# Moving the sums and roundings of Strassen operands T1 to T4 earlier at the batch boundaries of a fused attention and feed-forward kernel

## Chip, cores and metric

The kernel runs as one program on 1 core of a Trainium2 chip. The metric is its device time in microseconds, as the median of several runs; a lower time is better.

## What is computed

The reference is a linear attention, followed by two feed-forward layers. The change touches the first of them, `h = x @ w_in`, and what stands around it.

```python
# attention: q, k, v of (8 batches, 8 heads, 576 tokens, 64)
q_s = np.exp(q - np.max(q, axis=-1, keepdims=True))
q_s = q_s / (np.sum(q_s, axis=-1, keepdims=True) + 1e-09)
k_s = np.exp(k - np.max(k, axis=2, keepdims=True))
k_s = k_s / (np.sum(k_s, axis=2, keepdims=True) + 1e-09)
kv = np.einsum('bhsd,bhse->bhde', k_s, v)
x = np.einsum('bhsd,bhde->bhse', q_s, kv)        # then (4608 tokens, 512)
# first layer: w_in (512, 2048), w_out (2048, 512)
r = np.maximum(x @ w_in, 0.0)
x = (r * r) @ w_out
# second layer: rms norm, silu(xn @ w_gate) * (xn @ w_val) @ w_out
```

## The kernel before

**Products.** Every fp32 product is made of three matmuls in TensorE's round fp32 format: an operand is split in a rounded part ("hi", ScalarE, line 1116) and the rest ("lo", VectorE, line 1423, which reads the operand and its hi part). TensorE multiplies hi by hi, lo by hi and hi by lo (lines 1797 to 1799). The product `x @ w_in` of one batch (576 tokens, in two halves of 288) is a Strassen product: 7 products in place of 8. The four blocks of x are B11, B21 (first half of the tokens), B12, B22; the sums are T1 = B12 - B11, T2 = B22 - T1, T3 = B22 - B12 and T4 = B21 - T2. The seven operands of a batch are B11, T2, T1, B21, T3, T4, B22. GpSimd makes the sums: T1 at line 894 and T2 at line 899; T3 at line 902; T4 in two instructions, at lines 906 and 908, which overwrite the place in `xa` where T1 stands (so they wait until T1 is split). Batch 0 alone is computed as a plain product of four blocks; batches 1 to 7 go the Strassen way.

**Quads.** A batch has 8 quads (a quad is a pair of output blocks of 128 columns, times the two halves of the tokens), and a quad takes 7 steps on TensorE, one product (6 matmuls of 128x288) each. The order of the steps is B11, T2, T1, B21, then T4 and B22 of the quad before, then T3. All quads of a batch read the same seven operands in `TAR`, so operands are made once per batch, around the boundary between two batches. The tile `TAR` has 9 entries, so that most operands of a batch are written while those of the batch before are still read.

**Evacuation.** ScalarE copies the first product's bank (`h_copy_p1`, line 1157); TensorE adds B21 into that bank only after this copy (`pe.wait_ge(hp1_done, n)`). VectorE makes the other blocks: line 1471 (`h_u2`, which needs the copy, and for which T3 waits), 1476 (`h_21`), 1482 (`h_12`; the T1 product of the next quad but one waits for it), 1487 and 1489 (`h_22`).

**Attention beside it.** While a batch goes through the first layer, the attention of the next batch is computed in 4 units (c = 0 to 3), each a row of small tasks: `qmax` (VectorE, 1363), `qsub` (GpSimd, 882), `qexp` (ScalarE, 1070), `qsum` and `qinv` (VectorE, 1366 to 1373), `qnorm` (GpSimd, 885), then transposes of q (TensorE, 1786), the kv product (1771) and the x product (1790), with copies out of the banks by ScalarE (1086, 1090); kexp is at 1067, and kmax at 1358.

**The order.** Every engine runs its own list in order, with semaphore waits. The lists come from tables: `UNIT_*` give the steps of the attention's tasks, and `add_batches` adds, for each batch, splits and sums at step `start_of(b) + n - 56`, so n = 56 is the first step of batch b and n = 49 is the first step of the last quad of the batch before. Within a step the attention's tasks come first. The first unit of the batch after next to be computed has `qmax` at step 52, `qsub` and `kmax` at 53, `qexp` at 55, `qsum` at 56 and `qnorm` at 58 by the same count. The batch 7 boundary has no unit, since there is no batch 8.

```python
def ta_split(b, i):            # VectorE
    dve.wait_ge(ta_hi, split_a(b, i))
...
    if m == 0:                 # TensorE, the first quad of a batch
        pe.wait_ge(ta_lo, split_a(b, i))
...
elif which == T4 (the last branch of xa_sums, GpSimd):
    pool.wait_ge(ta_lo, split_a(b, T1))
```

`split_a` counts splits in the order of `SPLIT_A`.

Of the kernel before, what the change touches and what calls it, by code (L numbers as in the profile page):

```python
# [30 lines left out]
B11, T2, T1, B21, T3, T4, B22 = range(7)  # L31
# [20 lines left out]
NQA = B * PA  # L52
H_SETS = 3
W1_ALONE = 3
SPLIT_A = (B11, T2, T1, B21, T3, T4, B22)
SPLIT_PLAIN = (B11, B12, B21, B22)
PLAIN_ENTRY = {B11: 3, B12: 4, B21: 5, B22: 6}
BLOCKS = ((B11, B21), (B12, B22))
# [6 lines left out]
def start_of(b):  # L65
    return STEPS_PLAIN + STEPS * (b - 1) if b else 0
# [6 lines left out]
def split_a(b, i):  # L73
    return 4 + 7 * (b - 1) + SPLIT_A.index(i) + 1 if b else SPLIT_PLAIN.index(i) + 1

# [43 lines left out]
def unit_table(events):  # L119
    table = {}  # L120
    for b in range(1, B):
        for c in range(KC):
            base = start_of(b - 1) + UNIT_BASE[b - 1][c]
            for what, n in events:
                table.setdefault(max(0, base + n), []).append((what, b, c))
    return table


PE_AT, DVE_AT, ACT_AT, POOL_AT, SP_AT = (unit_table(t) for t in (UNIT_PE, UNIT_DVE, UNIT_ACT, UNIT_POOL, UNIT_SP))


def add_batches(table, what, at, second, later):
    for b in range(1, B):
        for i, n in at + (second if b == 1 else later):
            table.setdefault(start_of(b) + n - STEPS, []).append((what, b, i))


add_batches(ACT_AT, "split", [(B11, 28), (T2, 49), (T1, 51), (B21, 52), (T3, 55)], [(T4, 62), (B22, 64)], [(T4, 60), (B22, 63)])
add_batches(DVE_AT, "split", [(B11, 29), (T2, 50), (T1, 52), (B21, 53), (T3, 57)], [(T4, 64), (B22, 66)], [(T4, 62), (B22, 65)])
add_batches(POOL_AT, "sum", [(T1, 30), (T2, 47), (T3, 51)], [(T4, 60)], [(T4, 57)])  # L140
for _m in range(2, PA):
    ACT_AT.setdefault(8 * _m - 9, []).append(("w1", 0, _m))
    DVE_AT.setdefault(8 * _m - 8, []).append(("w1", 0, _m))
# [1930 lines left out]
```

## Time and profile before

| | |
|---|---|
| median of 3 runs | 1681.9 us (1679.25 to 1682.57) |
| the profiled execution | 1681.12 us |
| its span, first to last instruction | 1679.4 us |
| granted TensorE clock | 0.999 |
| TensorE busy (matmul) | 1652.1 us, 98% |
| VectorE busy | 1162.4 us, 69% |
| ScalarE busy | 615.1 us, 37% |
| GpSimd busy | 592.1 us, 35% |
| DMA queue's share of 16 engines | 41.6% |

The engines are called PE (TensorE), DVE (VectorE), ACT (ScalarE) and POOL (GpSimd) in the profile. A busy share is a mean over stages; what a stage is limited by is read from who waits for whom in that stage. The first Strassen layer lies between about 91 and 484 us, and its batches repeat every 56.4 us.

### The profile page before, as it was taken

The page shows a single profiled execution, that of the slowest core. Times are in us where ns is not written, and L with a number is a line of the kernel's source. Part 1 is how long each engine was busy: PE and PEld are TensorE (multiplying, and loading weights), DVE is VectorE, ACT ScalarE, POOL GpSimd, SP SyncE. Part 2 cuts the span into 40 slices and gives each one's busy share as a digit, 9 for nine tenths or more (in the row PEclk, how much of TensorE's full clock was granted, in tenths as well). Part 3 has the DMA queues.
Part 4 walks back from the last instruction along what each step waited for, and adds up shares of the span by engine and source line. Part 5 has one row for each costly group of instructions (what it writes and reads, how often), then busy time and mean ns, then how long its engine had stood idle before and what let it go on. Part 6 is the DMA issues. An engine that isn't in the chain of part 4 may idle for free.

```text
span 1679.4 us, 26396 instructions
## 1 busy us (share of the span) xinstructions
PE 1652.1 (98%) x9926; PEld 1510.5 (90%) x9926; DVE 1162.4 (69%) x1749; ACT 615.1 (37%) x1056; POOL 592.1 (35%) x470
## 2 busy tenths in 40 slices
PE   7999999999999999999999999999999998999999
PEld 6999999999988888888888988988998988999999
DVE  6687667667566778787776565546555568877775
ACT  5544334333232323333334432323332334343432
POOL 3553323332102224342256744546455553000000
PEclk9999999999999999999999999999999999999999
DMA  8665545554463454444432322242321334434441
GB/s 260 211 227 172 172 160 185 172 163 152 144 219 88 125 170 119 119 120 126 119 126 88 113 88 107 83 138 82 110 88 67 110 127 164 141 132 151 147 139 56
DMA packets 151742, 230.06 MB, mean 137 GB/s; under 512 B 11840, under 2 KB 75840, under 8 KB 151616
## 3 DMA queue, kind: packets, MB, share of 16 engines
q1 hardware_dynamic: 151616, 228.38, 41.6%
q8 instruction: 80, 1.31, 0.3%
q14 instruction: 46, 0.38, 0.1%
HBM read 143.39 MB, written 84.93 MB: 136 GB/s over the span
## 4 chain that ended last, share of the span: by engine, by line
PE 87%; DVE 6%; POOL 3%; DMA 2%; issue 1%; ACT 1%; SPq 0%; DVEq 0%; POOLq 0%; ACTq 0%
PE bank L1797 14%; PE bank L1798 14%; PE bank L1799 14%; PE bank L1883 7%; PE bank L1885 7%; PE bank L1884 7%; PE bank L1973 5%; PE bank L1975 5%; PE bank L1974 5%; PE bank L1771 2%; PE bank L1790 2%; DVE TAR L1423 1%; PE bank L1786 1%; DMA h_scratch<-hb 1%; PE bank L1818 1%
## 5 line engine op out<-in xcount | busy, mean ns | idle before, releaser
L1797 PE MATMUL bank<-TR,SW 128*128 128x512 f32 (+1 forms) x840 | 309.0, 368 | 0.3 <-DVE TR L1538 0.3
L1799 PE MATMUL bank<-TR,SW 128*128 128x512 f32 (+1 forms) x840 | 309.1, 368 | 0.0
L1798 PE MATMUL bank<-TR,SW 128*128 128x512 f32 (+1 forms) x840 | 309.1, 368 | 0.0
L1797 PE MATMUL bank<-TAR,SA 128*128 128x288 f32 x784 | 250.7, 320 | 5.5 <-DVE TAR L1423 2.8
L1798 PE MATMUL bank<-TAR,SA 128*128 128x288 f32 x784 | 231.5, 295 | 0.0
L1799 PE MATMUL bank<-TAR,SA 128*128 128x288 f32 x784 | 231.0, 295 | 0.0
L1883 PE MATMUL bank<-GH,W 128*128 128x512 f32 x576 | 224.7, 390 | 2.0 <-DVE GH L1443 2.0
L1885 PE MATMUL bank<-GH,W 128*128 128x512 f32 x576 | 224.5, 390 | 0.0
L1884 PE MATMUL bank<-GH,W 128*128 128x512 f32 x576 | 224.5, 390 | 0.0
L1132 ACT ACTIVATE GH<-g 128x512 fp32r<-128x512 f32 x144 | 91.2, 634 | 244.6 <-DVE g L1438 159.5
L1975 PE MATMUL bank<-SW,OA 128*128 128x256 f32 x630 | 179.3, 285 | 0.0
L1973 PE MATMUL bank<-SW,OA 128*128 128x256 f32 x630 | 179.3, 285 | 0.0
L1974 PE MATMUL bank<-SW,OA 128*128 128x256 f32 x630 | 179.3, 285 | 0.0
L1797 PEld LDWEIGHTS bank<-TR,SW 128*128 128x128 f32 x840 | 157.8, 188 | 20.5 <-DVE TR L1538 0.6
L1798 PEld LDWEIGHTS bank<-TR,SW 128*128 128x128 f32 x840 | 157.8, 188 | 19.8
L1799 PEld LDWEIGHTS bank<-TR,SW 128*128 128x128 f32 x840 | 157.8, 188 | 19.6
L1443 DVE TENSOR_TENSOR GH<-g,GH 128x512 fp32r<-128x512 f32 x144 | 138.7, 963 | 40.7 <-ACT GH L1132 40.6
L1797 PEld LDWEIGHTS bank<-TAR,SA 128*128 128x128 f32 x784 | 147.6, 188 | 10.5 <-DVE TAR L1423 4.6
L1798 PEld LDWEIGHTS bank<-TAR,SA 128*128 128x128 f32 x784 | 147.9, 189 | 2.5
L1799 PEld LDWEIGHTS bank<-TAR,SA 128*128 128x128 f32 x784 | 147.5, 188 | 0.0
L1013 POOL TENSOR_TENSOR group<-group,group 128x512 f32<-128x512 f32 (+1 forms) x60 | 73.0, 1216 | 189.9 <-DVE group L1584 189.5
L1883 PEld LDWEIGHTS bank<-GH,W 128*128 128x128 f32 x576 | 108.2, 188 | 25.1 <-DVE GH L1443 2.7
(176 smaller groups left out, 3344.0 us busy)
## 6 DMA issues: line engine op xcount, KB each, us to landing
h_scratch<-hb SPq DMA_DIRECT2D x128, 288.0 KB, 2.7
hst<-h_scratch SPq DMA_DIRECT2D x144, 256.0 KB, 2.7
araw<-a_scratch SPq DMA_DIRECT2D x18, 1536.0 KB, 6.8
a_scratch<-group SPq DMA_DIRECT2D x72, 256.0 KB, 2.0
xst<-xn_scratch SPq DMA_DIRECT2D x10, 1024.0 KB, 5.1
xn_scratch<-x SPq DMA_DIRECT2D x9, 1024.0 KB, 5.4
a_scratch<-group SPq DMA_DIRECT2D x48, 192.0 KB, 1.9
out<-ost SPq DMA_DIRECT2D x36, 256.0 KB, 2.0
```

The source lines that it names most:

```text
L1013: nc.gpsimd.tensor_tensor(a1, a1, val1, ALU.mult).then_inc(a1_done, 1)
L1132: nc.scalar.activation(GH[:, r % GH_RING, 0], g[:, r % G_RING], ACT.Copy).then_inc(ghi_done, 1)
L1443: nc.vector.tensor_tensor(GH[:, r % GH_RING, 1], g[:, r % G_RING], f(GH[:, r % GH_RING, 0]), ALU.subtract)\
L1797: nc.tensor.matmul(ps[:, 0:w], w_hi[:, cc], x_hi[:, c], start=opens and c == 0, stop=False, skip_group_check=True)
L1798: nc.tensor.matmul(ps[:, 0:w], w_lo[:, cc], x_hi[:, c], start=False, stop=False, skip_group_check=True)
L1799: last = nc.tensor.matmul(ps[:, 0:w], w_hi[:, cc], x_lo[:, c], start=False, stop=c == 1, skip_group_check=True)
L1883: nc.tensor.matmul(acc[c][:, :], W2[:, j, 0, cc], GH[:, r % GH_RING, 0], start=j == 0, stop=False, skip_group_check=True)
L1884: nc.tensor.matmul(acc[c][:, :], W2[:, j, 1, cc], GH[:, r % GH_RING, 0], start=False, stop=False, skip_group_check=True)
L1885: last = nc.tensor.matmul(acc[c][:, :], W2[:, j, 0, cc], GH[:, r % GH_RING, 1], start=False, stop=j == CA - 1, skip_group_check=True)
L1973: nc.tensor.matmul(ps, a_hi, w_hi, start=start, stop=False, skip_group_check=True)
L1974: nc.tensor.matmul(ps, a_lo, w_hi, start=False, stop=False, skip_group_check=True)
L1975: last = nc.tensor.matmul(ps, a_hi, w_lo, start=False, stop=stop, skip_group_check=True)
```

## The change

Three table lines and the tuple `SPLIT_A` change. T1 is split before T2 instead of after it. T4's two sums come directly behind T3's sum on GpSimd, ahead of the next unit's `qsub`; before, they came behind it. T3 and T4 are split at steps 53 and 54 of the old batch (ScalarE) and 54 and 55 (VectorE); before, at 55 and 60 (62 for batch 1), and 57 and 62 (64). No instruction is added or removed.

```diff
-SPLIT_A = (B11, T2, T1, B21, T3, T4, B22)
+SPLIT_A = (B11, T1, T2, B21, T3, T4, B22)
...
-add_batches(ACT_AT, "split", [(B11, 28), (T2, 49), (T1, 51), (B21, 52), (T3, 55)], [(T4, 62), (B22, 64)], [(T4, 60), (B22, 63)])
-add_batches(DVE_AT, "split", [(B11, 29), (T2, 50), (T1, 52), (B21, 53), (T3, 57)], [(T4, 64), (B22, 66)], [(T4, 62), (B22, 65)])
-add_batches(POOL_AT, "sum", [(T1, 30), (T2, 47), (T3, 51)], [(T4, 60)], [(T4, 57)])
+add_batches(ACT_AT, "split", [(B11, 28), (T1, 49), (T2, 51), (B21, 52), (T3, 53), (T4, 54)], [(B22, 64)], [(B22, 63)])
+add_batches(DVE_AT, "split", [(B11, 29), (T1, 50), (T2, 52), (B21, 53), (T3, 54), (T4, 55)], [(B22, 66)], [(B22, 65)])
+add_batches(POOL_AT, "sum", [(T1, 30), (T2, 47), (T3, 51), (T4, 52)], [], [])
```

GpSimd at the boundary to batch 2, before: T2's sum, T3's sum, `qsub`, T4's two sums, `qnorm`.

```order
L899 TENSOR_TENSOR TAR_106<-xa 128x576
L902 TENSOR_TENSOR xa<-xa 128x2x288
L882 TENSOR_TENSOR qn_113<-qn_113,qmax 128x640
L906 TENSOR_TENSOR xa<-xa 128x2x288
L908 TENSOR_TENSOR xa<-xa 128x2x288
L885 TENSOR_TENSOR qn_113<-qn_113,qinv 128x640
```

The same place after the change:

```order
L899 TENSOR_TENSOR TAR_106<-xa 128x576
L902 TENSOR_TENSOR xa<-xa 128x2x288
L906 TENSOR_TENSOR xa<-xa 128x2x288
L908 TENSOR_TENSOR xa<-xa 128x2x288
L882 TENSOR_TENSOR qn_113<-qn_113,qmax 128x640
L885 TENSOR_TENSOR qn_113<-qn_113,qinv 128x640
```

`qsub` (882) now stands behind both of T4's sums.

ScalarE at the same boundary, before: the evacuation copy of the old batch's last quad (1157), the splits of T2 (`TAR_106`) and T1, `h_11` (1164), the split of B21, `qexp` (1070), the split of T3, then the copy of the new batch's first quad, and the split of T4 behind `h_11`.

```order
L1157 ACTIVATE hb_0_126<-bank 128x288
L1116 ACTIVATE TAR<-TAR_106 128x576
L1116 ACTIVATE TAR<-xa 128x576
L1164 ACTIVATE hb_0_125<-bank 128x288
L1116 ACTIVATE TAR<-xa 128x576
L1070 ACTIVATE qn_113<-qn_113 128x640
L1116 ACTIVATE TAR<-xa 128x576
L1157 ACTIVATE hb_1_128<-bank 128x288
L1164 ACTIVATE hb_1_127<-bank 128x288
L1116 ACTIVATE TAR<-xa 128x576
```

After the change (the row with x3 is B21, T3 and T4):

```order
L1157 ACTIVATE hb_0_126<-bank 128x288
L1116 ACTIVATE TAR<-xa 128x576
L1116 ACTIVATE TAR<-TAR_106 128x576
L1164 ACTIVATE hb_0_125<-bank 128x288
L1116 ACTIVATE TAR<-xa 128x576 x3
L1070 ACTIVATE qn_113<-qn_113 128x640
L1157 ACTIVATE hb_1_128<-bank 128x288
L1164 ACTIVATE hb_1_127<-bank 128x288
```

T4's split now stands ahead of `qexp` and of the copy of the new batch's first quad.

VectorE from `kmax` (1358) of the same boundary to `h_u2` (1471) of the new batch's first quad and the rows behind it, before:

```order
L1358 TENSOR_REDUCE kmax<-kT_111 128x1
L1423 TENSOR_TENSOR TAR<-xa,TAR 128x576
L1482 TENSOR_TENSOR hb_2_129<-hb_2_129,bank 128x288
L1487 TENSOR_TENSOR hb_0_126<-hb_0_126,bank 128x288
L1489 TENSOR_TENSOR hb_0_126<-hb_0_126,bank 128x288
L1366 TENSOR_REDUCE qden<-qn_113 128x10
L1369 TENSOR_SCALAR qden<-qden 128x10
L1373 RECIPROCAL qinv<-qden 128x10
L1471 TENSOR_TENSOR hb_1_127<-hb_1_128,bank 128x288
L1423 TENSOR_TENSOR TAR<-xa,TAR 128x576
```

After the change:

```order
L1358 TENSOR_REDUCE kmax<-kT_111 128x1
L1423 TENSOR_TENSOR TAR<-xa,TAR 128x576
L1482 TENSOR_TENSOR hb_2_129<-hb_2_129,bank 128x288
L1423 TENSOR_TENSOR TAR<-xa,TAR 128x576
L1487 TENSOR_TENSOR hb_0_126<-hb_0_126,bank 128x288
L1489 TENSOR_TENSOR hb_0_126<-hb_0_126,bank 128x288
L1423 TENSOR_TENSOR TAR<-xa,TAR 128x576
L1366 TENSOR_REDUCE qden<-qn_113 128x10
L1369 TENSOR_SCALAR qden<-qden 128x10
L1373 RECIPROCAL qinv<-qden 128x10
L1471 TENSOR_TENSOR hb_1_127<-hb_1_128,bank 128x288
```

The lo splits of T3 and T4 moved from behind `h_u2` to ahead of `qsum` (1366) and `h_u2`.

## Rows read from the trace of the kernel before

**Rows 1.** The page's part 1: busy time, share and instructions by engine.

```profile
PE 1652.1 (98%) x9926; PEld 1510.5 (90%) x9926; DVE 1162.4 (69%) x1749; ACT 615.1 (37%) x1056; POOL 592.1 (35%) x470
```

**Rows 2.** Waits of PE: total us, times, longest us.

```profile
PE bank L1797 <- DVE TAR L1423: 2.8, 6, 0.5
```

**Rows 3.** Timeline of PE, boundary to batch 2: start, duration, [idle before <-releaser].

```profile
150.14 0.30 PE L1797 MATMUL bank<-TAR,SA 128*128 128x288 f32 x1
...
152.52 0.29 PE L1799 MATMUL bank<-TAR,SA 128*128 128x288 f32 x1
153.30 0.40 PE L1797 MATMUL bank<-TAR,SA 128*128 128x288 f32 x1 [0.49 <-DVE TAR L1423]
153.53 0.29 PE L1798 MATMUL bank<-TAR,SA 128*128 128x288 f32 x1
...
154.19 0.49 PE L1786 MATMUL bank<-ident,qn 128*128 128x128 f32 x3
```

**Rows 4.** Timeline of DVE, boundary to batch 2.

```profile
144.31 0.75 DVE L1423 TENSOR_TENSOR TAR<-TAR,TAR 128x576 fp32r<-128x576 f32 x1
...
145.71 0.75 DVE L1423 TENSOR_TENSOR TAR<-xa,TAR 128x576 fp32r<-128x576 f32 x1
146.38 0.45 DVE L1476 TENSOR_TENSOR hb<-hb,bank 128x288 f32<-128x288 f32 x1
146.74 0.74 DVE L1358 TENSOR_REDUCE kmax<-kT 128x1 f32<-128x576 f32 x1
147.41 0.79 DVE L1423 TENSOR_TENSOR TAR<-xa,TAR 128x576 fp32r<-128x576 f32 x1
...
149.34 0.81 DVE L1366 TENSOR_REDUCE qden<-qn 128x10 f32<-128x640 f32 x1
150.18 0.85 DVE L1369 TENSOR_SCALAR qden<-qden 128x10 f32<-128x10 f32 x1
...
151.20 0.43 DVE L1471 TENSOR_TENSOR hb<-hb,bank 128x288 f32<-128x288 f32 x1
151.55 1.69 DVE L1423 TENSOR_TENSOR TAR<-xa,TAR 128x576 fp32r<-128x576 f32 x1
```

**Rows 5.** Timeline of POOL, boundary to batch 2.

```profile
142.63 1.45 POOL L902 TENSOR_TENSOR xa<-xa 128x576 f32<-128x576 f32 x1
145.87 1.71 POOL L882 TENSOR_TENSOR qn<-qn,qmax 128x640 f32<-128x640 f32 x1 [1.79 <-DVE qmax L1363]
147.54 1.95 POOL L906 TENSOR_TENSOR xa<-xa 128x576 f32<-128x576 f32 x1
149.57 1.44 POOL L908 TENSOR_TENSOR xa<-xa 128x576 f32<-128x576 f32 x1
151.37 1.26 POOL L885 TENSOR_TENSOR qn<-qn,qinv 128x640 f32<-128x640 f32 x1 [0.36 <-DVE qinv L1373]
```

**Rows 6.** Timeline of ACT, boundary to batch 2.

```profile
147.62 0.74 ACT L1070 ACTIVATE qn<-qn 128x640 f32<-128x640 f32 x1 [1.09 <-POOL qn L882]
148.26 0.67 ACT L1116 ACTIVATE TAR<-xa 128x576 fp32r<-128x576 f32 x1
148.84 0.39 ACT L1157 ACTIVATE hb<-bank 128x288 f32<-128x288 f32 x1
```

**Rows 7.** Timeline of DVE, boundary to batch 1, and the stretch behind it.

```profile
92.89 0.17 DVE L1369 TENSOR_SCALAR qden<-qden 128x10 f32<-128x10 f32 x1
...
93.27 0.45 DVE L1471 TENSOR_TENSOR hb<-hb,bank 128x288 f32<-128x288 f32 x1
...
101.92 1.44 DVE L1423 TENSOR_TENSOR TAR<-xa,TAR 128x576 fp32r<-128x576 f32 x1
```

**Rows 8.** Timeline of PE behind the boundary to batch 1.

```profile
99.50 1.39 PE L1771 MATMUL bank<-vn,kt 128*128 128x129 f32 x10 [0.97 <-ACT qT L1086]
...
102.97 0.29 PE L1799 MATMUL bank<-TAR,SA 128*128 128x288 f32 x1
...
103.66 0.29 PE L1798 MATMUL bank<-TAR,SA 128*128 128x288 f32 x1
```

## The prediction

> **What bounds the kernel now.** I read the page first: TensorE is busy 98% of the span [rows 1], so only an idle stretch of TensorE can be won, and every new one is paid in full. The waits of PE come next. In the first layer the wait that this change can touch is the T3 product's for VectorE's lo split: 2.8 us in 6 waits [rows 2], one at each boundary to batches 1 to 6. Then the timelines of one boundary. PE's rows show what one wait costs: matmuls start every 0.13 us, so after 152.52 the second one of T3 was due at 152.78; it starts at 153.53, so 0.75 us is lost, 0.49 of it shown as idle [rows 3]. VectorE's rows show why: T3's lo split takes 1.69 us instead of 0.75 [rows 4], because `qnorm` runs on GpSimd from 151.37 to 152.63 [rows 5]. The split ends 0.61 us behind that.
>
> **The port rule that the rest uses.** An instruction of GpSimd and a lo split of VectorE do not run together. A split that meets a running GpSimd instruction ends 0.61 us after it (151.37 + 1.26 = 152.63; 151.55 + 1.69 = 153.24) [rows 4, 5]. A GpSimd instruction that meets a running split waits until about 0.64 us after the split's start: T4's first sum takes 1.95 instead of 1.44, so it truly begins at 148.05, against the split's start at 147.41 [rows 4, 5]. A split that had to wait frees the other 0.47 behind the instruction it waited for (I take 0.14 less than its end, as in the undisturbed one). VectorE's evacuations and reductions keep their durations beside GpSimd.
>
> The Trainium skill, page "SBUF — State Buffer", section "SBUF: two separate sides", says the same in sharper form: a VectorE operation with two SBUF inputs and a GpSimd operation that reads SBUF exclude each other, the first to start holds the port pair for its whole instruction. By that rule the pair would come free at 148.20 instead of 148.05; the row decides for the earlier release.
>
> **What the change removes.** T3's split moves ahead of `qnorm`, so the 0.75 us wait loses its cause at five boundaries (batches 2 to 6).
>
> **What it adds.** GpSimd runs T4's sums ahead of `qsub`, and ScalarE has T4's split, which waits for those sums, ahead of `qexp`, and both ahead of `h_copy_p1` of the new batch's first quad. TensorE's B21 product waits for that copy. I work the chain out for batch 2; up to the first lateness TensorE stands where it stands now.
>
> - T1's lo split takes the place of T2's: 144.31 to 145.06 [rows 4].
> - T4's first sum: 0.08 behind it (the gap between the two sums, 149.49 to 149.57), 145.14 to 146.59. T3's sum ended at 144.08, so GpSimd is free [rows 5].
> - T2's lo split starts at 145.71 [rows 4], meets this sum, and ends at 147.20, freeing the port at 147.06.
> - T4's second sum: due 146.67, begins at 147.06, ends at 148.50.
> - VectorE's next start is 147.13, 0.07 ahead of the end; 0.36 for line 1476 and 0.67 for `kmax` [rows 4] bring B21's lo split to 148.16. It meets the second sum, ends at 149.11, frees the port at 148.97.
> - `qsub`: 148.97 plus 1.26. That is its undisturbed duration (1.71 less the 0.45 during which the split of 145.71 held the port) [rows 4, 5]. It ends at 150.23.
> - `qexp`: 0.04 later, 150.27; the next ScalarE instruction starts 0.64 after it [rows 6], so the copy runs 150.91 to 151.32. Before it started at 148.84 [rows 6].
> - B21's first matmul was at 150.14 [rows 3]. Now 0.06 behind the copy, 151.38; the second follows a restart after 0.23, as at 153.30 to 153.53 [rows 3]: 151.61 against 150.27, so **1.34 us** is lost. The smaller lateness in front of it (`h_12` ends at 149.48, T1's product due at 149.34) lies inside this.
>
> What is late next: the `h_u2` for T3's product. VectorE after B21's split: `h_12` from 149.04, T3's split from 149.40. It meets `qsub`, which ends at 150.23, and so ends at 150.84. `h_22` (two instructions, 0.86 by starts: 149.34 less 147.41 is 1.93, less 0.71 for a split and 0.36) from 150.77; T4's split 151.63 to 152.38; `qsum` from 152.30 (0.84 to the next start, 149.34 to 150.18) [rows 4]; from line 1369 to `h_u2` 0.38, as 92.89 to 93.27 where nothing disturbs it [rows 7]. `h_u2` runs 153.52 to 153.97. T3's first matmul is at 154.03, the second at 154.26 against 152.78: **1.48 us** lost in all. Then `qnorm`, started 0.08 behind `qinv`'s end at 153.57, ends at 154.91; the transposes of q, which follow T3's first matmul by 0.89 (153.30 to 154.19) [rows 3], are due at 154.92. They come 0.05 to 0.15 late. I take 0.1: 1.58 us.
>
> **The sum.** At boundaries 2 to 6: 1.58 lost instead of 0.75, five times 0.83 = +4.2 us.
> At boundary 1 the same chain makes T3's product about 1.1 us later than before, but TensorE then waits 0.97 us for the copy of q [rows 8], which was late because T4's split stood ahead of it on ScalarE and waited for T4's sums. That wait goes as the other comes: taken together 0. B22's split (1.44 us [rows 7]) meets no `qsub` there any more, since the T4 sums no longer stand ahead on GpSimd; the product B22 lost 103.66 less 102.97 less 0.27 = 0.42 [rows 8]. So -0.4.
> At boundary 7 there is no unit, hence no `qsub` and no `qexp`: the copy would come 1.26 + 0.04 + 0.64 = 1.94 earlier than the 151.32 of the same place, at 149.38, which is ahead of 150.14. So 0.
> Total +3.8 us. The profiled execution took 1681.12 with a span of 1679.4; its span would be 1683.2. The median of before, 1681.9, is 0.8 above the profiled execution; with the same sum on it I predict **1685.7 us**. All later stages are as before, and move with TensorE. No DMA changes its place in SP's queue; at boundary 1 one store waits some 3 us longer for VectorE's copy, with loads behind it that are needed over 10 us later. I cost it at nothing.
>
> **Bounds.** From below: no sum meets a split. Then the sums end at 148.11, `qsub` at 149.30, the copy at 150.39, B21's second matmul at 150.68: 0.41 lost, 0.34 less than now, -1.7 us for five. With all that boundary 1 can give (0.97 + 0.42 = 1.4) it is -3.1: 1678.8. From above: each hold lasts the whole 0.75, three of them on the way to `qsub`, 0.42 a boundary, 2.1 in all, and boundary 1 gives nothing: 3.8 + 2.1 + 0.4 = +6.3: 1688.2. I stay with the release that the rows show.
>
> **Rivals.**
> - *The new wait is about as long as the old one.* For it: the port rule rests on few rows, and who gets the port first at 148.50 is not certain; any of the meetings at 145.71, 148.16 and 149.40 may fall away by a shift of some tenths. Result between -1.7 and +2.5 us, 1680.2 to 1684.4, about 1682.
> - *Faster.* T3's wait goes, and nothing takes its place: the copy at boundaries 2 to 6 ends before 150.08. It decides at `qsub`: this must end by 150.08 - 0.41 - 0.64 - 0.04 = 148.99. Against it: T4's two sums and `qsub`, 1.45 + 0.08 + 1.44 + 1.26 less 0.07 of overlap, take 4.16 us from 145.14 even without any meeting, and end at 149.30. For it: spans on GpSimd are rough, and 0.31 is little. Price: 5 x 0.75 + 1.4 = 5.1 us, 1676.8.
> - *The port is held longer*, or the late `h_u2` makes later quads late too (`h_12` and `h_21` of the old batch's last quad follow it on VectorE): 0.42 more a boundary, 1687.8. Against it: T4's split is no longer in the way there, and the rows of before have idle VectorE soon after. By the page's rule the whole instruction holds the pair, which is this case; the trace shows an earlier release.
>
> **How the numbers follow.** A measurement of this kernel can tell about 0.2%, 3.4 us, from no change. Forecast, +2.5 to +5.5: 0.52, of which 0.35 above +3.4. New wait like the old: 0.20. Faster: 0.13 (1676.8, or less of it, but past -3.4). Longer hold: 0.15. Slower by over 0.2% is 0.35 + 0.15 = 0.50; within, 0.17 + 0.20 = 0.37; faster 0.13. The range 1678.8 to 1688.5 takes in both bounds and leaves out most of the faster case and the tail above.
>
> **What would show it.** In the profile of the changed kernel: no wait of line 1797 for TAR's lo split at boundaries 2 to 6; in its place a wait of the B21 product for line 1157, about 1 us each, and one of some tenths for line 1471 or 885. `qexp` at 150.3 by the same clock, ScalarE idle ahead of T4's split for line 908. At boundary 1 no wait of line 1771 for qT. The period of batches 57.3 us instead of 56.4. Wrong would be: `qsub` ending near 149.3 (no meetings at the port), or a wait of T2's or B21's product for its split, which I have as on time by 1.3 and 1.0 us.

## The result, and the profile after

The changed kernel takes 1685.47 us (median of 12 runs, 1684.47 to 1686.70), the kernel before 1681.76 us in runs beside it (median of 12). The ratio is 1.0025, with a 95% interval of 1.0018 to 1.0033: slower by 0.25%, or 3.7 us. 1685.7 was predicted.

The page's part 1 of the changed kernel, against [rows 1]. TensorE's share is 98% as before, and the page does not show the loss. One reason is that a matmul is recorded as 0.29 us long while the next starts 0.13 us behind it, so a start that is a little late leaves no gap in the record and counts as busy. The losses are therefore read from starts.

```profile
PE 1656.9 (98%) x9926; PEld 1512.3 (90%) x9926; DVE 1165.0 (69%) x1749; ACT 615.7 (37%) x1056; POOL 590.6 (35%) x470
```

The waits of PE (total us, times, longest us). The wait of line 1797 for TAR's lo splits [rows 2] is gone; the list now begins with the copy.

```profile
PE bank L1797 <- ACT hb L1157: 6.0, 8, 1.0
...
PE bank L1797 <- DVE hb L1471: 1.0, 1, 1.0
```

PE's timeline at the boundary to batch 2, against [rows 3]. The clock of this execution is 0.19 us ahead of the other's here (the copy of the old batch's last quad starts at 143.33 instead of 143.14), so 0.19 is to be taken off every time of the changed kernel at this boundary.

```profile
150.49 0.29 PE L1799 MATMUL bank<-TAR,SA 128*128 128x288 f32 x1
151.62 0.37 PE L1797 MATMUL bank<-TAR,SA 128*128 128x288 f32 x1 [0.83 <-ACT hb L1157]
151.82 0.30 PE L1798 MATMUL bank<-TAR,SA 128*128 128x288 f32 x1
...
154.05 0.29 PE L1799 MATMUL bank<-TAR,SA 128*128 128x288 f32 x1
154.23 0.37 PE L1797 MATMUL bank<-TAR,SA 128*128 128x288 f32 x1
154.43 0.29 PE L1798 MATMUL bank<-TAR,SA 128*128 128x288 f32 x1
...
155.22 0.52 PE L1786 MATMUL bank<-ident,qn 128*128 128x128 f32 x3
```

The second matmul of B21 is at 151.82 - 0.19 = 151.63 instead of 150.27 (lost: 1.36), the second of T3 at 154.24 instead of 152.78 (lost: 1.46). T3's wait is too short for the view to name, but its first matmul starts 0.18 us behind the last one, where 0.13 is the pace. GpSimd's timeline shows where the time is lost, against [rows 5]:

```profile
145.33 1.43 POOL L906 TENSOR_TENSOR xa<-xa 128x576 f32<-128x576 f32 x1 [1.07 <-DVE TAR L1423]
146.84 1.83 POOL L908 TENSOR_TENSOR xa<-xa 128x576 f32<-128x576 f32 x1
148.64 1.77 POOL L882 TENSOR_TENSOR qn<-qn,qmax 128x640 f32<-128x640 f32 x1
153.81 1.26 POOL L885 TENSOR_TENSOR qn<-qn,qinv 128x640 f32<-128x640 f32 x1 [3.41 <-DVE qinv L1373]
```

Two of the four are stretched (1.83 and 1.77, against 1.44 and 1.26 undisturbed), and VectorE's timeline shows the lo splits that they meet, each stretched too (0.75 undisturbed), against [rows 4]:

```profile
145.90 1.48 DVE L1423 TENSOR_TENSOR TAR<-TAR,TAR 128x576 fp32r<-128x576 f32 x1
...
148.32 0.96 DVE L1423 TENSOR_TENSOR TAR<-xa,TAR 128x576 fp32r<-128x576 f32 x1
...
149.57 1.45 DVE L1423 TENSOR_TENSOR TAR<-xa,TAR 128x576 fp32r<-128x576 f32 x1
...
153.31 0.17 DVE L1369 TENSOR_SCALAR qden<-qden 128x10 f32<-128x10 f32 x1
...
153.65 0.43 DVE L1471 TENSOR_TENSOR hb<-hb,bank 128x288 f32<-128x288 f32 x1
```

ScalarE's timeline, against [rows 6]: T4's split waits for the second sum, `qexp` for `qsub`, and the copy stands behind both. It starts 2.05 us later than before (151.08 - 0.19 against 148.84).

```profile
148.70 0.69 ACT L1116 ACTIVATE TAR<-xa 128x576 fp32r<-128x576 f32 x1 [1.42 <-POOL xa L908]
150.44 0.74 ACT L1070 ACTIVATE qn<-qn 128x640 f32<-128x640 f32 x1 [1.05 <-POOL qn L882]
151.08 0.39 ACT L1157 ACTIVATE hb<-bank 128x288 f32<-128x288 f32 x1
```

**Period.** A transpose of kmax (line 1774) comes with each of the four units of a batch. The one of the first unit stands directly behind B21's product of the new batch's first quad, so the distance of its starts in batches 2 and 6, divided by 4, gives the period of the batches to some hundredths of a microsecond. That is finer than the spread of the runs. PE's timeline of the kernel before:

```profile
150.94 0.27 PE L1774 MATMUL bank<-ident,kmax 128*128 128x128 f32 x1
```

The same of the changed kernel:

```profile
152.48 0.27 PE L1774 MATMUL bank<-ident,kmax 128*128 128x128 f32 x1
```

In batch 6 they start at 376.72 and 381.75. The periods are 56.45 and 57.32: 0.87 us more at each boundary.

**Boundary 1.** PE's timeline behind it, against [rows 8]: T3 waits 0.97 us for `h_u2`, and the kv product (line 1771), which waited 0.97 for the copy of q before, no longer waits.

```profile
96.92 0.37 PE L1797 MATMUL bank<-TAR,SA 128*128 128x288 f32 x1 [0.97 <-DVE hb L1471]
...
100.10 1.39 PE L1771 MATMUL bank<-vn,kt 128*128 128x129 f32 x10
```

From batch 1's first matmul (91.47 before, 91.91 after) to the second unit's kmax transpose (106.86 and 107.05), which lies behind all of this, it is 15.39 us before and 15.14 after, so -0.25.

### The profile page after: what moved, and what is told of

It is laid out like the page before. It is cut to its first block, busy times and chain, and to the rows that moved or that the text cites. A ratio compares the mean times of both kernels' runs of the same rounds, so it can differ in the third digit from the quotient of the medians.

```text
span 1684.1 us, 26396 instructions
## 1 busy us (share of the span) xinstructions
PE 1656.9 (98%) x9926; PEld 1512.3 (90%) x9926; DVE 1165.0 (69%) x1749; ACT 615.7 (37%) x1056; POOL 590.6 (35%) x470
## 4 chain that ended last, share of the span: by engine, by line
PE 90%; DVE 3%; POOL 3%; DMA 1%; issue 1%; ACT 1%; SPq 0%; ACTq 0%; DVEq 0%; POOLq 0%
PE bank L1797 15%; PE bank L1798 15%; PE bank L1799 15%; PE bank L1883 7%; PE bank L1885 7%; PE bank L1884 7%; PE bank L1973 5%; PE bank L1975 5%; PE bank L1974 5%; PE bank L1771 2%; PE bank L1790 2%; PE bank L1786 1%; DMA h_scratch<-hb 1%; PE bank L1819 1%; PE bank L1818 1%
```

## The experiments

Times are medians; each ratio is to the kernel before in runs made beside it (median 1681.34 us for e1 to e4, 1681.64 for e5, e7, e8 and e9, 1681.18 for e10). Periods are worked out as above, from the kmax transposes of batches 2 and 6:

```
kernel                                   batch 2   batch 6   period   median us   ratio to before (95%)
before                                    150.94    376.72    56.45    1681.76
changed                                   152.48    381.75    57.32    1685.47     1.0025 (1.0018-1.0033)
e1  T3 early alone                        150.09    373.73    55.91    1678.49     0.9981 (0.9972-0.9990)
e2  changed, T4 split late                153.25    381.43    57.05    1684.69     1.0017 (1.0008-1.0026)
e3  T1 before T2 alone                    150.74    376.54    56.45    1681.46     0.9999 (0.9990-1.0009)
e4  changed, copy ahead of qexp           151.99    381.25    57.32    1685.62     1.0025 (1.0016-1.0034)
e5  changed, half of T4's sums            149.88    376.28    56.60    1679.95     0.9993 (0.9984-1.0002)
e7  changed, half of B21's lo split       152.51    380.59    57.02    1684.48     1.0018 (1.0009-1.0027)
e8  changed, e2 and e4 together           152.14    378.74    56.65    1682.08     1.0005 (0.9996-1.0014)
e9  e1, and T4 behind q's copy at 1       149.20    372.89    55.92    1677.69     0.9978 (0.9969-0.9987)
e10 e9, and T4's sums behind qnorm        149.81    373.29    55.87    1676.89     0.9972 (0.9962-0.9983)
```

Two theories were stated. Theory A is the prediction's: T4's sums make `qsub`, `qexp` and the copy late, and `h_u2` and `qnorm` are late right behind. Theory B: the loss is VectorE's alone, which has lo splits ahead of `qsum` and `h_u2`.

**T3 early alone (e1).** The kernel before with one part of the change.

```diff
-ACT: ..., (B21, 52), (T3, 55)]     DVE: ..., (B21, 53), (T3, 57)]
+ACT: ..., (B21, 52), (T3, 53)]     DVE: ..., (B21, 53), (T3, 54)]
```

> The kernel before, with one part of the change: T3's splits at steps 53 (ScalarE) and 54 (VectorE); T4's sums stay behind qsub and T4's splits stay late, T2 stays ahead of T1. Theory A (the change lost through the chain T4 sums, qsub, qexp, copy of the first quad, with h_u2 and qnorm right behind it): here nothing stands ahead of qsub, so qexp starts at its old place and the copy is on time. T3's lo split meets T4's first sum instead of qnorm (ends about 150.10 by the clock of batch 2), h_u2 ends about 152.56, just ahead of T3's product at 152.65. The wait of 0.75 us goes at five boundaries; at boundary 1 the wait for the copy of q stays. 3.3 to 3.8 us faster than the kernel before: about 1678.2, and no wait of line 1797 for TAR from boundary 2 on. Theory B (the loss is VectorE's: lo splits ahead of qsum and h_u2 make h_u2 late): T3's split ahead of h_u2 shows a wait for line 1471 instead, about as long as the old one; 1681 to 1683.

1678.49 us, 2.9 us faster than before; no wait for TAR's lo splits from boundary 2 on. VectorE's timeline at the boundary to batch 2 (this clock is 0.85 behind that of the kernel before):

```profile
147.63 1.61 DVE L1423 TENSOR_TENSOR TAR<-xa,TAR 128x576 fp32r<-128x576 f32 x1
...
151.20 0.43 DVE L1471 TENSOR_TENSOR hb<-hb,bank 128x288 f32<-128x288 f32 x1
```

T3's split meets T4's first sum, as expected, and `h_u2` ends at 151.63, 0.17 us ahead of T3's product (151.80). The period falls by 0.54, not by 0.67 to 0.75: `qnorm` ends about 0.2 us late for q's transposes. At boundary 1 the wait only moved: the kv product waits 1.52 us for q's copy, where it waited 0.97. So the wait that the change removes is worth 2.7 us, and the change's other parts cost more than twice as much. For T3's split theory B fails here: this lo split ahead of `h_u2` brings no wait at all. T4's split is not tested by this run; e2 and e8 do that.

**T4's splits late (e2).** The changed kernel, sums early, splits at the old steps.

```diff
-ACT: (T3, 53), (T4, 54)], [(B22, 64)], [(B22, 63)]      DVE: (T3, 54), (T4, 55)], [(B22, 66)], [(B22, 65)]
+ACT: (T3, 53)], [(T4, 62), (B22, 64)], [(T4, 60), (B22, 63)]      DVE: (T3, 54)], [(T4, 64), (B22, 66)], [(T4, 62), (B22, 65)]
```

> The changed kernel with T4's splits back at their old late steps (ScalarE 60 and 62, VectorE 62 and 64); T4's sums stay ahead of qsub on GpSimd. Theory A: qsub is as late as in the changed kernel, so the wait of B21 for the copy stays at 0.8 us of idle time; VectorE's T4 split (0.67) is gone from ahead of h_u2, so the second lateness (1.48 less 1.34, and qnorm's 0.1) goes: 0.24 a boundary, 1.2 us faster than the changed kernel, about 1684.3. Theory B: h_u2 loses 0.67 of its lateness and with it most of the loss goes, 1681 to 1682.5. A third reading, that T4's split blocks ScalarE's queue ahead of the copy by itself: the copy is then on time and the time 1681 or less.

1684.69 us; the period is 0.27 below the changed kernel's, where 0.24 was expected, and the copy's wait is unchanged. PE's timeline, boundary to batch 2:

```profile
152.38 0.37 PE L1797 MATMUL bank<-TAR,SA 128*128 128x288 f32 x1 [0.84 <-ACT hb L1157]
```

T4's split on ScalarE is therefore not what holds the copy; `qsub` is. Theory B fails in the whole as well: with T4's split gone from ahead of `h_u2` it wanted 1681 to 1682.5 us.

**T1 before T2 alone (e3).** The kernel before with T1 and T2 exchanged.

```diff
-SPLIT_A = (B11, T2, T1, B21, T3, T4, B22)      ACT: (T2, 49), (T1, 51)      DVE: (T2, 50), (T1, 52)
+SPLIT_A = (B11, T1, T2, B21, T3, T4, B22)      ACT: (T1, 49), (T2, 51)      DVE: (T1, 50), (T2, 52)
```

> The kernel before, with only T1 and T2 exchanged in the order of splits on ScalarE and VectorE (and in the count that TensorE waits for). Theory A and B: T2's product waits for a split that ends at about 146.5, two microseconds ahead; nothing changes, 1681.8 within 1 us. The rival, that this exchange is part of the loss: over 1683.

1681.46 us, period 56.45. This part costs nothing.

**The copy ahead of `qexp` (e4).** The changed kernel, with `qexp` of the first unit one step later on ScalarE.

```diff
+for _n, _b in [(start_of(_b - 1) + UNIT_BASE[_b - 1][0] - 7, _b) for _b in range(2, B)]:
+    ACT_AT[_n].remove(("qexp", _b, 0)), ACT_AT.setdefault(_n + 1, []).insert(0, ("qexp", _b, 0))
```

> The changed kernel with the first unit's qexp one step later on ScalarE at boundaries 1 to 6, behind the copy of the new batch's first quad. Theory A in its two links: the copy no longer waits for qsub, and starts about 0.35 us behind its old place, so the wait of B21's product for line 1157 vanishes. But h_u2 still stands behind T3's and T4's lo splits and qsum, which needs the same qexp; T3's product then takes over the whole wait, about 1.2 us idle for line 1471, 1.5 us lost. The time stays within 1 us of the changed kernel: 1684.5 to 1686. If the copy's wait were the whole cause, this kernel would be 1.3 x 5 us faster than the changed one: 1679.

1685.62 us: no gain, though the wait that heads the changed kernel's list is gone. PE's timeline, boundary to batch 2:

```profile
154.80 0.38 PE L1797 MATMUL bank<-TAR,SA 128*128 128x288 f32 x1 [0.93 <-DVE hb L1471]
```

(About 1.2 us of idle time was expected there. This clock is 0.76 ahead of that of the kernel before, so T3's product starts at 154.04 as in the changed kernel.)

ScalarE's timeline of the same kernel shows the copy ahead of `qexp`, which waits for `qsub` as before:

```profile
149.87 0.39 ACT L1157 ACTIVATE hb<-bank 128x288 f32<-128x288 f32 x1
151.01 0.74 ACT L1070 ACTIVATE qn<-qn 128x640 f32<-128x640 f32 x1 [0.75 <-POOL qn L882]
```

The idle time moved from B21's product to T3's, and the period is the same to 0.01 us. Two latenesses of nearly one size (1.36 and 1.46) stand one behind the other; taking away the first uncovers the second.

**Both (e8).** The changed kernel with the edits of e2 and e4.

> The changed kernel with both: qexp of the first unit behind the copy (as in the run that did this alone) and T4's splits late. The two links of the chain are both shortened: no wait for the copy, and h_u2 0.67 us earlier than in the run with the copy ahead. 0.8 us lost per boundary at T3's product (idle for line 1471 about 0.3 to 0.5), against 0.75 in the kernel before: about 1681.5, 3.8 us below the changed kernel, though either edit alone gave 1.2 or nothing. If the links add up instead (1.2 + 0 = 1.2), it is 1684.3.

1682.08 us; the period is 0.67 below the changed kernel's, against 0.27 and 0.00 for the two edits alone. PE's timeline, boundary to batch 2:

```profile
154.28 0.37 PE L1797 MATMUL bank<-TAR,SA 128*128 128x288 f32 x1 [0.26 <-DVE hb L1471]
```

Together the edits give more than twice their sum: the 0.67 us of VectorE's time that T4's split took ahead of `h_u2` pays in full only once the copy is out of the way, and the copy's place pays only once `h_u2` is earlier.

**Half of T4's sums (e5).** The changed kernel; the other half of T4 is left uncomputed.

```diff
+                    b11, b21, b22 = (t[:, :, 0:TA // 2] for t in (b11, b21, b22))
                     nc.gpsimd.tensor_tensor(b11, b22, b11, ALU.subtract).then_inc(xa_sum, 1)
```

> The changed kernel with T4's two sums over half of their columns (144 of 288 in each block; the other half of T4 is left wrong), so each takes about 0.8 us instead of 1.44. Chain theory, worked out again from the same rows: second sum ends about 1.3 us earlier than in the changed kernel, qsub and qexp with it, so the copy is on time and B21's wait for line 1157 is gone at boundaries 2 to 6. h_u2 is still some 0.5 us late (it stands behind T3's and T4's splits and qsum): a wait for line 1471 of about 0.4 us, 0.7 to 0.8 us lost instead of 1.58. Time 4.1 us below the changed kernel, about the time before: 1681 to 1682. Rival, that the order on ScalarE (T4's split ahead of qexp) costs by itself, whatever the sums take: stays above 1684.

1679.95 us. The period is 0.72 below the changed kernel's, where 0.8 was expected. The order on ScalarE is that of the changed kernel, and no wait for the copy is left when the sums are short. What remains against e1 (56.60 against 55.91) goes with `h_u2`, ahead of which T4's lo split still stands. GpSimd's timeline, boundary to batch 2 (this clock is 1.33 behind that of the kernel before):

```profile
143.81 0.81 POOL L907 TENSOR_TENSOR xa<-xa 128x288 f32<-128x288 f32 x1 [1.06 <-DVE TAR L1424]
144.70 1.21 POOL L909 TENSOR_TENSOR xa<-xa 128x288 f32<-128x288 f32 x1
145.87 1.26 POOL L882 TENSOR_TENSOR qn<-qn,qmax 128x640 f32<-128x640 f32 x1
```

PE's timeline of it:

```profile
151.98 0.37 PE L1798 MATMUL bank<-TAR,SA 128*128 128x288 f32 x1 [0.25 <-DVE hb L1472]
```

The median is 1.5 us below the middle of what was expected: 1.2 us were also won at boundary 1 (13.94 us from batch 1's first matmul, 91.59, to the second unit's kmax transpose at 105.53, against 15.14), which the expectation left out.

**Half of B21's lo split (e7).** The changed kernel; from batch 2 on half of this rest is left uncomputed.

```diff
+                w = TA // 2 if b >= 2 and i == B21 else TA
```

(`w` then bounds the columns of the lo split's three operands.)

> The changed kernel with VectorE's lo split of B21 over half of its columns from batch 2 on (the rest keeps old values). Port rule: the split that meets T4's second sum holds the port 0.23 us less, so qsub's duration in the timeline falls from 1.77 to about 1.53 us, and qexp, the copy, T3's lo split and h_u2 all come 0.23 earlier; the period of batches falls from 57.31 to about 57.08, 1.2 us off the changed kernel: 1684.3. If qsub's long duration has another cause (spans on GpSimd are rough), qsub stays at 1.77 and the period at 57.3.

1684.48 us; `qsub` falls from 1.77 to 1.48 us, and the period by 0.30, where 0.23 was expected. The split itself is shorter by 0.30 (0.66 against 0.96). GpSimd's timeline, boundary to batch 2:

```profile
148.95 1.48 POOL L882 TENSOR_TENSOR qn<-qn,qmax 128x640 f32<-128x640 f32 x1
```

VectorE's (the edits of e5 and e7 shift the later lines by one, so that the lo split is 1424):

```profile
148.65 0.66 DVE L1424 TENSOR_TENSOR TAR<-xa,TAR 128x288 fp32r<-128x288 f32 x1
```

A shorter instruction on VectorE makes an instruction on GpSimd shorter that shares neither data nor a semaphore with it. Spans on GpSimd that are merely rough would not do this.

**The version that beats both (e9).** e1, and at batch 1 ScalarE's T4 split one step later, behind the first copy of q.

```diff
-ACT: [(T4, 62), (B22, 64)], [(T4, 60), (B22, 63)]
+ACT: [(T4, 63), (B22, 64)], [(T4, 60), (B22, 63)]
```

> The faster version: the kernel before with T3's splits early at all batches, and at batch 1 alone ScalarE's T4 split behind the first copy of q (step 63 instead of 62). At boundary 1 TensorE's kv product waits 1.5 us for that copy, which stands behind T4's split, which waits for T4's sums; with the exchange the copy of q starts when h_copy_p1 and the transposes are done. 1.0 to 1.5 us below the version without it (1678.5): about 1677.3; the wait of line 1771 for qT gone or under 0.3. Rival: the wait passes to B22's or T4's product of that quad, gain under 0.5.

1677.69 us: 3.9 us faster than before (ratio 0.9978) and, by the two ratios, 0.47% faster than the changed kernel. Its interval overlaps e1's, and its period is e1's (55.92 and 55.91), so the gain over e1 shows only at boundary 1: no wait for q's copy is left, and from batch 1's first matmul (91.08) to the second unit's kmax transpose (105.13) it is 14.05 us, against e1's 15.31. A wait for B22's lo split at boundary 1, seen in the kernel before too, grew (PE's timeline):

```profile
101.66 0.40 PE L1797 MATMUL bank<-TAR,SA 128*128 128x288 f32 x1 [0.54 <-DVE TAR L1423]
```

**T4's sums behind `qnorm` (e10).** e9 with T4's sums at step 60 at every batch, T4's splits at 63 and 64, B22's at 64 and 66.

> The fastest version so far (T3's splits early; at batch 1 ScalarE's T4 split behind the first copy of q), with T4's sums behind qnorm on GpSimd at every batch, as batch 1 has them, and T4's and B22's splits at batch 1's steps. At boundaries 2 to 6 of the version before it, T3's lo split meets T4's first sum and takes 1.61 us, and the second sum then delays nothing but leaves qinv and qnorm 0.2 us late for q's transposes. Here no sum runs there: T3's lo split takes 0.75, qnorm starts about 0.85 earlier, and the 0.2 us go: period 55.7 instead of 55.92, 1 us below the version before it, about 1676.6. Rival: T4's and B22's lo splits now meet qnorm's successors (the sums, and qsub of the second unit), the product B22 waits 0.1 to 0.5 us as it does at batch 1, and the period stays at 55.9 or rises to 56.2.

1676.89 us, the fastest, but its interval overlaps e9's, and the period fell by 0.05 only, not by 0.2. q's transposes do start 0.19 earlier behind the kmax transpose (2.50 us instead of 2.69). Most of that is given back at B22's product. VectorE's timeline behind the boundary to batch 2:

```profile
157.34 0.76 DVE L1423 TENSOR_TENSOR TAR<-xa,TAR 128x576 fp32r<-128x576 f32 x1
```

PE's:

```profile
158.15 0.40 PE L1797 MATMUL bank<-TAR,SA 128*128 128x288 f32 x1
158.39 0.30 PE L1798 MATMUL bank<-TAR,SA 128*128 128x288 f32 x1
```

The split ends at 158.10, the product starts at 158.15, 0.20 behind the matmul before it, and its second matmul comes 0.24 behind the first. Both steps are 0.13 otherwise, so 0.18 us is lost: the rival of that expectation, in small.

## Why the prediction was right

- **The wait of T3's product goes.** Shown: none is left, and the part of the change that removes it gives 2.9 us when it is made alone (e1).
- **The chain over `qsub`.** Each step came within 0.06 us of its forecast once the 0.19 are taken off: T4's second sum ends at 148.48 (148.50 forecast), `qsub` at 150.22 (150.23), the copy starts at 150.89 (150.91), B21 has lost 1.36 (1.34). That the sums' length is the cause, and not the place of T4's split on ScalarE, is shown by e2 and e5.
- **The port rule** (a lo split of VectorE and an instruction of GpSimd do not run together). Three meetings were forecast and three occurred, so the rival that needed one of them to fall away failed. The split that met `qsub` took 1.45 us, one that meets nothing 0.75. e7 shows the rule in the other direction. The rule left one case out: the small VectorE instruction of line 1369, recorded as 0.85 us at 150.18 in [rows 4], ends 0.02 us behind GpSimd's second T4 sum (149.57 + 1.44 = 151.01), and takes 0.17 where no GpSimd instruction runs (153.31 above). So it seems to wait as well, which no run tests; in the kernel before it stands ahead of `h_u2` and T3's split with 0.68 us more. The forecast took its undisturbed spacing for the changed kernel, where nothing meets it, and this did no harm. The split's hold on a waiting GpSimd instruction is the early release that the rows showed: T4's second sum started at 146.84 and, with 1.44 of its own, truly at 147.23, while T2's split ended at 147.38. The sharper rule of the Trainium skill, page "SBUF — State Buffer", section "SBUF: two separate sides" (the pair is held for the whole instruction), would have it begin at 147.38; the trace puts the release 0.15 earlier. That two such operations exclude each other, as that page of the Trainium skill says, the trace bears out.
- **`h_u2`.** Forecast 1.48 lost at T3, measured 1.46. e4 shows that this lateness stands by itself behind the copy's, e8 that both have to go.
- **`qnorm`.** Forecast 0.1 us, and 0.13 measured at the transposes (155.22 - 154.43 = 0.79 behind T3's second matmul, against 0.66 in [rows 3]). Whether all of it reaches the end is open: of 0.19 us of the same kind e10 kept 0.05, with a new wait at B22.
- **The sum.** Forecast five times 0.83 and -0.4 at boundary 1; measured five times 0.87 and -0.25, which is 4.1 us against the 3.8 forecast. At boundary 1 B22's 0.42 went as forecast, but T3's lateness and the old wait for q's copy did not cancel exactly: the kv product starts 8.03 us behind batch 1's first matmul before and 8.19 after. At boundary 7 nothing was forecast, and 0.04 us is lost.
- **Luck in the total.** The median agrees with 1685.7 to 0.2 us, and the structure was 0.3 us off, so part of this agreement is chance. The two profiled executions differ by 4.7 us, of which 0.44 lie ahead of batch 1. From batch 6's kmax transpose to the second layer's first matmul (line 1883) the changed kernel takes 101.61 us against 103.08, where the last boundary with a unit accounts for 0.5 less (0.65 less at T3, 0.13 more at q's transposes), and from there to the end 1200.74 against 1199.60. e4, with the changed kernel's period, has 103.45 and 1199.10, so these stretches scatter by more than 1 us from one execution to another.
- **What was overlooked.** At boundary 1 I took the old wait for q's copy as simply exchanged for T3's. That is nearly what happened, but it hid a gain of over 1 us for whoever removes both (e9).
- **The rivals.** The faster case failed where it was said to be decided: `qsub` ended at 150.22, not by 148.99. The longer hold did not occur.

## What to carry to other kernels

When an engine in the middle of a dependency chain gets work inserted, follow its queue through every engine to the product that waits, and then look for the next product that waits for the same engines: the wait at the head of the list (here 0.83 us for the copy) was worth nothing alone, because 1.46 us of lateness stood behind it. A change made of several moves should be timed move by move: one of these three gave 2.9 us (e1), one nothing (e3), and the third, moving T4's sums and splits, took more than the first gave. No run makes the third alone; its cost is the difference of the periods of the changed kernel and e1, 1.41 us a boundary. Where VectorE's splits and GpSimd's instructions can meet, cost them by who meets whom, not by their undisturbed durations.

## What the runs showed of the hardware

- The two directions differ in the rows: a lo split that waits for a GpSimd instruction ends 0.61 us behind it (151.02 against 150.41 in the changed kernel), and a GpSimd instruction that waits for a split goes on 0.13 to 0.15 before the split's recorded end. Halving the split's columns (e7) shortened the GpSimd instruction that waits for it by 0.29 us.
- The first matmul of batch 1's Strassen products started between 90.71 us (e1) and 92.70 us (e2) in the profiled executions of kernels that do the same up to the last few microseconds in front of it. This scatter of 2 us comes from ahead of the changed part. As much lies behind it: from batch 6's kmax transpose to the second layer's first matmul it takes between 101.21 us (e10) and 103.51 us (e1). There ScalarE's copies wait for stores of `hb`, the longest in e1 (ScalarE's timeline):

```profile
459.00 0.41 ACT L1157 ACTIVATE hb<-bank 128x288 f32<-128x288 f32 x1 [5.96 <-DMA h_scratch<-hb]
```

Both are about as large as the effects measured. Periods of the repeated batches repeat to 0.01 us (56.45 in the kernel before and in e3, 57.32 in the changed kernel and in e4), so they separate kernels that medians do not.
